# An attention and two mixture-of-experts layers on one core: GpSimd drained ahead of the last scatters, the output cleared behind the flags' gather

## The reference

```python
# 1. retention: 2 batches x 8 heads x 768 steps, head width 64
state = gamma * state + outer(k[t], v[t]);  y[t] = q[t] @ state / 8
x = y as (1536, 512)
# 2. first expert layer, 8 experts 512 -> 1024 -> 512, top-1 gate, rows with x @ w_skip <= 0 pass through
x[row] += gate * relu(x[row] @ w1[e]) @ w2[e]
# 3. second expert layer, top-1, each expert takes its first `capacity` (384) rows in row order
out = 0
out[row] = gate * relu(x[row] @ w1[e]) @ w2[e]      # kept rows only; the others stay zero
```

## Time and profile before

| what | value |
|---|---|
| median of 3 runs | 401.75 us |
| the profiled execution's own time | 401.38 us |
| its span in the profile | 399.5 us |
| PE busy | 382.5 us (96%) |
| DVE / ACT / POOL busy | 260.5 / 171.1 / 84.2 us |
| granted clock of PE, mean over the span | 0.993 |

### The profile page before, as it was taken

How to read it: one execution, slowest core, us unless ns; L and a number is a source line. 1 busy time by engine, 2 the same in 40 slices (tenths; PEclk the granted TensorE clock), 3 DMA queues, 4 the chain that set the end, 5 groups by cost and what they waited for, 6 DMA issues and landing times.

```text
span 399.5 us, 7617 instructions
## 1 busy us (share of the span) xinstructions
PE 382.5 (96%) x2863; PEld 343.1 (86%) x2863; DVE 260.5 (65%) x462; ACT 171.1 (43%) x217; POOL 84.2 (21%) x82
## 2 busy tenths in 40 slices
PE   8999998999999999999799999999999999999990
PEld 6888887799889988997688988989989898998980
DVE  2886787859989888976496467363654736365420
ACT  2445443514432454252354445455444545544410
POOL 4110000421443412231700330403003040300100
PEclk9999999999999999999999999999999999999997
DMA  8999997499999999438299967766747676610100
GB/s 268 368 378 384 345 329 242 104 354 396 390 390 387 390 386 376 155 132 318 84 370 394 381 201 251 230 211 230 258 138 264 208 229 199 224 63 0 52 26 8
DMA packets 55858, 101.02 MB, mean 253 GB/s; under 512 B 6661, under 2 KB 18437, under 8 KB 55696
## 3 DMA queue, kind: packets, MB, share of 16 engines
q1 hardware_dynamic: 46048, 85.67, 60.2%
q0 software_dynamic: 4416, 11.18, 8.2%
q10 hardware_dynamic: 5360, 3.70, 3.1%
HBM read 89.39 MB, written 12.73 MB: 256 GB/s over the span
## 4 chain that ended last, share of the span: by engine, by line
PE 85%; DMA 6%; DVE 2%; issue 2%; SPq 2%; ACT 1%; POOL 1%; DVEq 0%; ACTq 0%; POOLq 0%
PE ps_h L1359 36%; PE ps_y L1385 28%; PE ps_r L1247 3%; PE ps_o L1234 3%; PE ps_s L1199 3%; PE ps_y L1401 3%; PE ps_t L1330 2%; PE ps_u L1213 2%; PE ps_o L1226 2%; DMA fits<-flags,slot_row 2%; DMA flags<-fits 2%; DMA iw<-in_consts 1%; PE ps_h L1186 1%; DMA xg<-x_rows,slot_in 1%; PE ps_t L1422 0%
## 5 line engine op out<-in xcount | busy, mean ns | idle before, releaser
L1006 DVE TENSOR_TENSOR w_lo<-raw,w_hi 128x2048 fp32r<-128x2048 f32 x48 | 109.0, 2287 | 23.2 <-ACT w_hi L706 20.5
L706 ACT CAST w_hi<-raw 128x2048 fp32r<-128x2048 f32 x48 | 90.4, 1904 | 4.4 <-PE ps_y L1385 2.6
L1017 DVE SCALAR_TENSOR_TENSOR h_lo<-ps_h,h_hi 128x512 fp32r<-128x512 f32 x48 | 32.9, 688 | 60.9 <-ACT h_hi L715 60.9
L1385 PE MATMUL ps_y<-w_hi,h_hi 128*128 128x512 f32 x176 | 70.8, 402 | 0.0
L715 ACT ACTIVATE h_hi<-ps_h 128x512 fp32r<-128x512 f32 x48 | 28.7, 597 | 94.5 <-PE ps_h L1359 94.5
L1385 PE MATMUL ps_y<-w_hi,h_lo 128*128 128x512 f32 x176 | 68.8, 391 | 0.0
L1385 PE MATMUL ps_y<-w_lo,h_hi 128*128 128x512 f32 x176 | 68.7, 390 | 0.0
L1359 PEld LDWEIGHTS ps_h<-x_f,raw 128*128 128x128 f32 x512 | 58.4, 192 | 1.3 <-issue 0.7
L1359 PE MATMUL ps_h<-x_f,raw 128*128 128x128 f32 x512 | 58.7, 275 | 0.3 <-ACT x_f L711 0.3
L1359 PE MATMUL ps_h<-x_hi,w_hi 128*128 128x256 f32 x256 | 41.3, 284 | 0.3 <-ACT x_hi L711 0.2
L1359 PE MATMUL ps_h<-x_lo,w_hi 128*128 128x256 f32 x256 | 41.2, 283 | 0.0
(11 more groups left out here) (164 smaller groups left out, 428.1 us busy)
## 6 DMA issues: line engine op xcount, KB each, us to landing
raw<-in_moe_w SPq DMA_DIRECT2D x64, 1024.0 KB, 8.1
q_t<-in_q_cols SPq DMA_DIRECT2D x16, 192.0 KB, 6.3
k_t<-in_k_cols SPq DMA_DIRECT2D x16, 192.0 KB, 6.3
x_rows<-rows ACTq DMA_DIRECT2D x8, 384.0 KB, 4.8
k_in<-in_k_rows SPq DMA_DIRECT2D x15, 192.0 KB, 6.4
v_in<-in_v_rows SPq DMA_DIRECT2D x15, 192.0 KB, 6.4
out<-zero SPq DMA_DIRECT2D x1, 2816.0 KB, 19.9
w_wide<-w_next SPq DMA_DIRECT2D x1, 2048.0 KB, 14.3
```

The lines of the kernel that those rows point to most:

```text
L706: nc.scalar.copy(w_hi[c], raw[:, 4 * job.par + c, :]).then_inc(hi_done[c], 1)
L1006: nc.vector.tensor_tensor(w_lo[c], raw[:, 4 * job.par + c, :], w_hi[c].bitcast(F32), ALU.subtract).then_inc(lo_done[c], 1)
L1017: nc.vector.scalar_tensor_tensor(out=h_lo[:, cols], in0=ps_h[:, g % 2, :], scalar=0.0, in1=h_hi[:, cols].bitcast(F32), op0=ALU.max, op1=AL ...
L1385: last = pe.matmul(ps_y[:, t, :], ht, wt, start=(fb == 0 and z == 0), stop=(fb == 2 * QB - 1 and z == 2))
```

## The change

Two edits. The first is in SP's program: the two clearing DMAs wait for `flags_in` (both gathers of the flags have landed) where they waited for the first turn of the second layer. The second is in POOL's: in the second layer a DRAIN stands between the scatter of job 6 and that of job 7.

```diff
@@ -485,7 +485,7 @@
                 if layer.i == 1:
                     hold(sp, lg2_in, n_win * 16)
                     load_pair(0, first=True)
-                    sp.wait_ge(turned[1], 1)
+                    hold(sp, flags_in, 16 * LATE)
                     sp.dma_start(out[P // 2:P, :], zero[P // 2:P, 0:DM]).then_inc(out_cleared, 16)
                     sp.dma_start(out[P:N, :].rearrange("(g p) d -> p g d", p=P), repeat(zero[:, 0:DM], 1, G - 1)).then_inc(out_cleared, 16)
                 n_win = windows(sp, layer)
@@ -601,6 +601,8 @@
                                 bounds_check=N - 1, oob_is_err=False).then_inc(flags_in, 16)
                     for e in range(E - 1):
                         step(Job(layer, base, w, e // 2, e % 2))
+                    if i == 1:
+                        pool.drain()
                     scatter(Job(layer, base, w, E // 2 - 1, 1), by_block=i == 1)
```

## The result

The changed kernel takes 396.0 us (median of 4, 395.41 to 396.06) against 401.8 us for the kernel before on the same chip (401.65 to 402.5): a ratio of 0.9849 [0.9832, 0.9866], 5.8 us. Forecast were 397.1 us, range 395.7 to 399.8. A second series gave 395.64 against 401.02, 0.9863 [0.9849, 0.9878]. The profiled execution is one of 395.41 us with a span of 393.6.

A forecast was written before the change was run, and what follows sets the result against it. PE bounds the kernel, busy 382.5 of 399.5 us; open are 5.5 us of closing DRAIN and a 0.57 us gap at 231. 401.38 − 5.07 + 0.4 = 396.7, plus 0.37 for the median: 397.1 us, range 395.7 to 399.8.

The forecast's parts named there:

- The closing DRAIN has a price for each of POOL's DMAs: POOL's end: DRAIN settles 66 DMAs at 80 ns each; with two left it falls from 5.47 to 0.4 us.
- my three arguments: On the closing DRAIN's 5.5 us: it waits for no data, has no fixed price, and queue upkeep is not paid at issue.
- The rule that I weighed: A drain waits for its engine to go fully idle; by that alone the DRAIN part is 0, forecast about 402.
- The DRAIN by hand is hidden: POOL after job 6's scatters: 5.3 us from 371.2, inside 14.18 us of idle time, over 6 us to spare.
- The flags come 8 us earlier, and the gap goes: Ahead of `map_final`: flags land at 222.4 instead of 230.42, PE's 0.57 us gap goes, 0.5 us gained.
- The gather of job 2 comes late: POOL's gather, issued at 236.7, takes 7.1 us among full queues; PE waits some 0.9 us at the turn near 243.
- Rival (c): Job 2's gather lands among the loads in under 6.1 us: 396.2 us; lower part of the own case, together 0.75.
- edit 2: SP's clears moved behind the flags' gather: 0.5 us gained, 0.9 lost at job 2's turn, net 0.4 us lost.
- edit 1: POOL's DRAIN ahead of job 7's scatters: 5.07 us off the closing DRAIN, all on the path; bounds 0 and 5.3.
- (a): Closing DRAIN's price is fixed once POOL has issued any DMA, so moving it gains 0: 402.1 us; chance 0.14.
- (b): DRAIN's price has both parts, or a bounded number of DMAs is held, so half goes: 399.5 us; chance 0.05.
- (d): Moved queue holds up job 2's gather by 17.6 us, PE stands 11.3 us at the turn: 407.5 us; chance 0.06.

The follow-up runs named there:

- the kernel with 58: Kernel before the change plus one DRAIN on POOL right behind its first eight DMAs, 58 behind it: 400.25 against 401.04 us, 0.9983.
- Edit 1 alone: Changed kernel with the clears put back to wait for the second layer's first turn, DRAIN ahead of job 7's scatters kept: 395.68 against 401.18 us, 0.9861.
- edit 2 alone: Changed kernel without the DRAIN, clears still behind the flags' gather: 400.38 us, 0.9978.
- the doubled clear: Changed kernel with a second clear of 2816 KB into a spare DRAM tensor, right behind the first in SP's queue: 399.53 against 401.04 us, 0.9961.

## Why the prediction was right

**The closing DRAIN has a price for each of POOL's DMAs: right.** It was worked out from two rows of one trace, 66 DMAs at 80 ns; the five counts of DMAs above give 82 ns and a base of 58. The 188 ns of the earlier trace rows, which I took as the base, is not that: POOL's first memsets ran until 0.46 us under that DRAIN, which opened at 0.32. So the remainder was 0.22 us, not 0.4, and the term −5.24, not −5.07. That only the second layer's DMAs might be open is excluded by the kernel with 58. One of my three arguments was weaker than it reads: the scatter at 118.72 is POOL's 18th DMA and not some 25th, and others before the last took 1.5 to 3.1 us to make, so the two equal 0.97 us were chosen rows. The experiments carry the reading, not that argument. The rule that I weighed, from the Trainium skill, PSUM — Partial Sum Buffer, section Engine vs sequencer instructions, agrees with what the DRAINs did first, which lasted at least until POOL had made its descriptors; it doesn't explain 5465 ns on a POOL that had nothing under way.

**The DRAIN by hand is hidden: right, its length off.** Forecast 5.3 us at 371.2; recorded 7.2 from 368.5 to 375.79. The part behind the last scatter's issue is 375.79 − 370.48 = 5.31 us, and 58 + 64 × 82 ns = 5.31 us. The further wait for that scatter's landing, 1.6 us, for which I had left room, did not come: in a second trace of the same kernel it landed 1.7 us into this stretch (372.38), and the DRAIN lasted no longer. The cover was 14.18 us, of which over 6 were to be left; 8.9 were left (375.79 to 384.67).

**The flags come 8 us earlier, and the gap goes: right, its worth under-read.** In at 221.7, forecast 222.4. I took the gap's 0.57 less the step between instructions, 0.5. PE won 0.75. The waits view of the kernel before has PE's weight load idle for longer than the gap:
```profile
PEld ps_e L1298 <- DVE final L1090: 0.8, 1, 0.8
```
A gap in front of a matmul counts from the recorded end of the last one. In a row without a gap the next group starts before that end: 0.16 us before it at `map_final` in the changed kernel (230.73 against 230.25 + 0.64). This overlap is lost beside the gap: 0.57 + 0.16 = 0.73 us. Edit 1 alone has a gap of 0.49, so 0.65, and needs 0.65 us more for this stretch than the changed kernel (12.73 against 12.08).

**The gather of job 2 comes late: wrong.** This is the step that failed. I took "7.1, the mean of the two that met a full queue", and so a stall of 0.9 us. It landed in 6.25, the turn started at once, and what is left is 0.11 us. The full load was there (share 1.02), and the issue at 236.50, forecast 236.7; the latency alone was off. Six traces of kernels with the clears behind the flags' store or gathers record its landing, at 6.15 to 6.21 us. It is tempting to put the 7.2 us of the earlier trace rows down to the clear issued at 201.90, beside which that gather partly ran. The record says no: with the clears 15 to 20 us later the same gather of job 1 still needs 6.8 to 7.5 us. In the trace of edit 2 alone (DMA issues, 198.9 to 199.6 us):
```profile
xg<-x_rows,slot_in POOLq DMA_INDIRECT x1, 7.1
```
The flags' second gather, 7.07 us, ran from 223.35 on beside loads too, and the first of that pair took 5.3. Part of the difference is POOL's own: making the descriptors took 2.45 us for the flags' second gather and 1.00 for the one of job 2. So full queues of loads gave 5.3 to 7.5 us for one of these gathers, the stall began at about 6.3, and a mean of two high rows decided a question that their scatter left open. Why the gather of job 1 needs a microsecond more than that of job 2 in the same queues is open. Rival (c), "in under 6.1 us", described what happened, though at 6.25. So edit 2 gave 0.64 us where I had 0.4 lost, which with the drain's 0.17 makes up the 1.1 us between forecast and result. By the prediction's own last sentence, a gap of PE that is not there near 243, this half of the forecast was wrong; the total fell into the range since edit 1 carries nine tenths of it.

**The rivals.** (a), a fixed price, and (b), half of it, are excluded by the line through five counts. (d), a gather held up by the backlog to beyond 11.7 us, is excluded for this kernel; the doubled clear shows a stall of that kind (8.7 us, PE stands for 2.35), yet not of the size of a chunk on SP's own queue, 17.6 us.

## What to carry to other kernels

Look at what the engines do behind the last work. In this kernel the DRAIN on GpSimd that closes it costs 82 ns for each DMA that GpSimd issued since the last DRAIN, and a DRAIN by hand in an idle stretch of GpSimd moves that cost to where nobody waits for it. A long chain through DMAs costs the gap that it leaves on the busy engine and the small overlap lost with it, not its length. When bulk writes are moved, ask for each small transfer what it then runs beside, and who waits for it: here a small load that came later moved SP's own bulk loads onto a scatter on which the next layer waits. And when a change is worth less than the spread of the times, compare the stretch that it can alter, from landmark to landmark.

## What was unexpected of the hardware

A DRAIN of GpSimd with all its DMAs landed takes 58 + 82 × n ns, n being its DMAs since the last DRAIN, within 10 ns for 2, 12, 28, 58 and 66 (222, 1038, 2345, 4804 and 5465 ns); for 1 it took 120. Placed right behind DMAs it begins while they are in flight (3.19 and 5.31 us for 38 and 64, as by the line), and where they land late it ends behind the landing (10.8 us in one place). Indirect gathers of GpSimd needed 2.4 to 3.3 us with the DMA engines empty, 5.3 to 8.0 beside SP's loads into SBUF at full rate, and 6.6 to 8.7 beside SP's clearing writes into DRAM. These include 1.0 to 3.1 us in which GpSimd makes the descriptors, the last two ranges overlap, and no run tells the direction from the amount.
